# Spread in one tile width; token rows written early in three transfers, gates in a table of their own with a second gather per tile

## The reference, cut to what matters

```python
# _moe_ref: logits = x @ phi; slot_input = softmax_over_rows(logits).T @ x
slot_out[e] = relu(slot_input[e] @ w1[e]) @ w2[e]
x = softmax_over_slots(logits) @ slot_out          # comb @ slot_out
# _moe2_ref:
logits = x @ w_gate; e_idx = argmax(logits, axis=1)
gate_w = softmax(logits)[n, e_idx]
eom = sigmoid(x @ w_output_gate)
out[mask_e] = gate_w * eom[:, e] * (relu(x[mask_e] @ v1[e]) @ v2[e])
```

## Time and profile before

| | |
|---|---|
| median of 3 runs | 523.88 us (521.13 to 524.0) |
| profiled execution | 524.51 us, of it span 522.8 |
| mean granted TensorE clock | 0.959 |
| TensorE busy | 464.9 us, 89% of the span |
| L859, output products | 249.2 us |
| DMA queue of SP | 77.27 MB, 41.5% of 16 engines' time |

### The profile page before, as it was taken

The page is one execution under the profiler, slowest core; times in us unless marked ns, Lnnn a source line. Parts: engine busy times, 40 slices in busy tenths (PEclk is TensorE's granted clock), DMA queues, the critical chain, the costliest instruction groups (busy, mean ns, idle before and its releaser), DMA issues.

```text
span 522.8 us, 10083 instructions
## 1 busy us (share of the span) xinstructions
PE 464.9 (89%) x3524; PEld 253.7 (49%) x3525; DVE 135.9 (26%) x278; ACT 144.4 (28%) x330; POOL 139.4 (27%) x206
## 2 busy tenths in 40 slices
PE   4788886799847997889999999999999999999991
PEld 3567664553205444365454554554545545445440
DVE  1389899820000667110010110101101001011000
ACT  2587774301000343322121221211212212122110
POOL 2144433056000121402322323223233232232210
PEclk9999999899885798799999999999999999999997
DMA  8869736849999977876786101011011010110110
GB/s 253 278 228 322 260 101 230 319 173 369 387 390 409 396 270 291 257 239 192 243 291 222 44 26 46 26 43 43 26 46 43 26 46 23 45 43 23 41 42 2
DMA packets 42690, 88.35 MB, mean 169 GB/s; under 512 B 6142, under 2 KB 15362, under 8 KB 42656
## 3 DMA queue, kind: packets, MB, share of 16 engines
q1 hardware_dynamic: 37616, 77.27, 41.5%
q0 software_dynamic: 3952, 10.33, 5.9%
q10 hardware_dynamic: 1088, 0.26, 0.2%
HBM read 77.61 MB, written 10.59 MB: 169 GB/s over the span
## 4 chain that ended last, share of the span: by engine, by line
PE 78%; DVE 9%; DMA 4%; issue 3%; ACT 3%; SPq 0%; POOL 0%; DVEq 0%; POOLq 0%; ACTq 0%
PE bank L859 47%; DMA arena<-in_moe_w 4%; PE bank L848 3%; PE bank L847 3%; PE bank L722 3%; PE bank L523 3%; PE bank L740 2%; PE bank L515 2%; ACT parts L996 2%; PE bank L770 2%; PE bank L534 2%; DVE rsum L1103 1%; PE bank L787 1%; PE bank L789 1%; PE bank L788 1%
## 5 line engine op out<-in xcount | busy, mean ns | idle before, releaser
L859 PE MATMUL bank<-arena,z 128*128 x560 | 249.2, 598 | 1.0 <-DVE z L1367 0.8
L859 PEld LDWEIGHTS bank<-arena,z 128*128 128x128 f32 x560 | 103.6, 190 | 122.0 <-issue 119.9
L1367 DVE TENSOR_SCALAR z<-bank 128x512 f32<-128x512 f32 x35 | 24.2, 691 | 251.8 <-PE bank L848 251.8
L1034 ACT ACTIVATE z<-bank,tile_gate 128x512 f32<-128x512 f32 x35 | 24.0, 687 | 227.8 <-PE bank L859 227.8
L454 POOL COPY rows_to<-sidx 128x1 int32 (+1 forms) x35 | 6.3, 181 | 152.4 <-ACT z L1034 152.4
L462 POOL DMA_INDIRECT z<-token_rows,rows_from x36 | 37.9, 1054 | 29.0 <-POOL rows_from L454 29.0
L472 POOL DMA_INDIRECT out<-z,rows_to x35 | 35.7, 1019 | 29.9 <-POOL rows_to L454 29.9
L847 PE MATMUL bank<-cT,parts 128*128 128x128 bf16 x280 | 36.4, 219 | 0.5 <-issue 0.5
L848 PE MATMUL bank<-cT,parts 128*128 128x128 bf16 x280 | 36.5, 219 | 0.1
L847 PEld LDWEIGHTS bank<-cT,parts 128*128 x280 | 27.4, 98 | 1.2 <-issue 0.9
L848 PEld LDWEIGHTS bank<-cT,parts 128*128 x280 | 27.4, 98 | 1.0 <-issue 0.5
(11 more groups left out here) (223 smaller groups left out, 497.6 us busy)
## 6 DMA issues: line engine op xcount, KB each, us to landing
arena<-in_moe_w SPq DMA_DIRECT2D x31, 2048.0 KB, 11.6
arena<-in_x SPq DMA_DIRECT2D x8, 1024.0 KB, 7.2
parts<-in_moe_w SPq DMA_DIRECT2D x1, 2048.0 KB, 9.2
token_rows<-z SPq DMA_DIRECT2D x8, 162.0 KB, 3.2
z<-token_rows,rows_from POOLq DMA_INDIRECT x36, 2.6
out<-z,rows_to POOLq DMA_INDIRECT x35
z<-in_state ACTq DMA_DIRECT2D x4, 64.0 KB, 3.0
z<-in_state SPq DMA_DIRECT2D x4, 64.0 KB, 2.7
```

The source lines that it names most:

```text
L859: mm = e.matmul(pY[p][:, :], hT[p][:, c, :], arena[:, bass.ds(ex * UNIT + 512 * c, 512)], start=(c == 0), stop=(c == CF - 1))
L1034: e.activation(ysb[p], pY[p][:, :], ACT.Copy, scale=tile_gate[:, q:q + 1])\
L1367: e.tensor_scalar(hT[p][:, 4:8, :], bank[2 * p + 1][:, :].rearrange("p (c t) -> p c t", c=4), 0.0, None, ALU.max).then_inc(relu_v, 1)
```

## The change

- `spread` uses stationary operands of 64 columns throughout. `pick` has zeros in its outer two blocks, so that [I I], [I 0] and [0 I] can be cut from it; the upper half of banks 0 and 1 is a sum of two matmuls. 20 matmuls per expert in place of 16, 12 for banks 0 and 1 first, and a semaphore `spread_a` after them. ACT waits for `spread_a` for banks 0 and 1 and for `spread_psum` for banks 2 and 3; TensorE waits for ga_ready ahead of the first group and for gb_ready ahead of the second.
- The row table is 80 words wide and written after load 11 instead of load 20, in three DMAs of SP, as soon as GpSimd's copy is done.
- The gates go to a table of their own, by three DMAs issued by ACT after part_2(1). GpSimd gathers a tile's gates by a second indirect DMA into `tile_gate`; ACT's copy L1018 and its waits go.
- GpSimd's step is scatter(t), then gather(t+4) and gather_gate. The v2 loads of experts 0 and 1 no longer wait for gathers.

```diff
-            for u in range(8, 21):
+            for u in range(8, 12):
                 load_w(u)
-
-            e.wait_ge(row_ready, 2)
-            for b in range(NB):
-                e.dma_start(table[b * (S + NS):b * (S + NS) + S, :].rearrange("(p j) w -> p j w", j=J),
-                            rowbuf[:, J * b:J * b + J, :]).then_inc(table_out, 16)
-                q, f = b % 4, b // 4
-                e.dma_start(table[b * (S + NS) + S:(b + 1) * (S + NS), :],
-                            rowbuf[32 * q:32 * q + 32, NB * J + f, :]).then_inc(table_out, 16)
-            for u in range(21, NU):
+            e.wait_ge(row_ready, 1)
+            by_batch = table.rearrange("(b r) w -> b r w", b=NB)
+            e.dma_start(by_batch[:, 0:S, :].rearrange("b (p j) w -> p b (j w)", j=J),
+                        rowbuf[:, 0:NB * J, :].rearrange("p (b j) w -> p b (j w)", b=NB)).then_inc(table_out, 16)
+            for f in range(2):
+                e.dma_start(by_batch[4 * f:4 * f + 4, S:S + NS, :],
+                            rowbuf[:, NB * J + f, :]).then_inc(table_out, 16)
+            for u in range(12, NU):
                 load_w(u)
...
-                if ex < 2:
-                    e.wait_ge(gathers, 2 * ex + 2)
-                else:
+                if ex >= 2:
...
+            def gather_gate(q):
+                e.sem_inc(gate_turns, 1)
+                e.indirect_dma_start(tile_gate[:, q:q + 1], None, gates,
+                                     bass.IndirectOffsetOnAxis(ap=rows_from[:, q:q + 1], axis=0),
+                                     bounds_check=last_row, oob_is_err=False).then_inc(gate_in[q], 16)
...
             def step(t, q, first=False):
+                scatter(t, q, first and t < 2)
                 with live_tile(e, live, t + 4):
                     if not isinstance(t, int) or t + 4 < ST:
                         gather(t + 4, q)
-                scatter(t, q, first and t < 2)
+                        gather_gate(q)
...
-                gather(t, t, first=True)
+                gather(t, t)
+            e.wait_ge(gates_out, 16 * 3)
+            for t in range(4):
+                gather_gate(t)
...
                 if ex >= 1:
                     e.wait_ge(ga_ready, 2 * ex)
+                for q in range(4):
+                    at, cols = half(q)
+                    e.matmul(bank[q // 2][0:64, cols], at[:, 32:96], g1, start=True, stop=True)
+                    e.matmul(bank[q // 2][64:P, cols], at[:, 64:P], g1, start=True, stop=False)
+                    mm = e.matmul(bank[q // 2][64:P, cols], at[:, 0:64], g2, start=False, stop=True)
+                mm.then_inc(spread_a, 1)
+                if ex >= 1:
                     e.wait_ge(gb_ready, 2 * ex)
-                g1, g2, g3 = gp[ex % 2]
                 for q in range(4):
...
-                    e.matmul(ba[0:96, cols], at[:, 0:96], g1, start=True, stop=True)
-                    e.matmul(ba[96:P, cols], at[:, 0:32], g2, start=True, stop=True)
-                    e.matmul(bb[0:64, cols], at[:, 0:64], g2, start=True, stop=True)
-                    mm = e.matmul(bb[64:P, cols], at[:, 0:64], g3, start=True, stop=True)
+                    at, cols = half(q)
+                    e.matmul(bank[2 + q // 2][0:64, cols], at[:, 32:96], g2, start=True, stop=True)
+                    mm = e.matmul(bank[2 + q // 2][64:P, cols], at[:, 32:96], g3, start=True, stop=True)
                 mm.then_inc(spread_psum, 1)
...
+            e.wait_ge(gate_ready, 1)
+            by_batch = gates.rearrange("(b r) w -> b r w", b=NB)
+            e.dma_start(by_batch[:, 0:S, :].rearrange("b (p j) w -> p b (j w)", j=J),
+                        gate[:, 0:NB * J].rearrange("p (b j) -> p b j", b=NB)).then_inc(gates_out, 16)
+            for f in range(2):
+                e.dma_start(by_batch[4 * f:4 * f + 4, S:S + NS, :],
+                            gate[:, NB * J + f:NB * J + f + 1]).then_inc(gates_out, 16)
...
-                if not isinstance(t, int) or t > 3:
-                    e.wait_ge(y_copied, t - 3)
-                e.activation(tile_gate[:, q:q + 1], row[q][:, GATE_W:GATE_W + 1], ACT.Copy).then_inc(gate_saved, 1)
...
+                e.wait_ge(gate_in[q], 4 * (t - q) + 16)
...
-            e.wait_ge(row_ready, 1)
-            e.tensor_tensor(rowbuf[:, :, GATE_W], gate[:, :], st1[:, :], ALU.mult).then_inc(row_ready, 1)
+            e.tensor_tensor(gate[:, :], gate[:, :], st1[:, :], ALU.mult).then_inc(gate_ready, 1)
```

More of the change, by code:

```diff
@@ L40 @@
 UNIT = CD * F
-ROWW = 81
-GATE_W = 80
+ROWW = 80
 NOROW = 1 << 20
@@ L53, in last_user, with build @@
     return before[-1] if before else None
-def build(nc, x, state, phi, w1, w2, wgate, wogate, v1, v2, out, table):
+def build(nc, x, state, phi, w1, w2, wgate, wogate, v1, v2, out, table, gates):
     with ExitStack() as ctx:
@@ L221, in build @@
                                                        sem("sidx_ready"))
+        pick_zero = sem("pick_zero")
         pick_ready, table_out, row_zero = sem("pick_ready"), sem("table_out"), sem("row_zero")
@@ L229, in build @@
         y_psum, y_copied, from_copied, to_copied = sem("y_psum"), sem("y_copied"), sem("from_copied"), sem("to_copied")
-        gate_saved = sem("gate_saved")
+        gates_out, gate_in, gate_turns = sem("gates_out"), [sem(f"gate_in{q}") for q in range(4)], sem("gate_turns")
+        gate_ready = sem("gate_ready")
         turns, gathers, scatters = sem("turns"), sem("gathers"), sem("scatters")
@@ L390, in _ @@
             e.wait_ge(consts, 3)
+            e.memset(pick[:, :, :, :], 0.0).then_inc(pick_zero, 1)
+            e.wait_ge(pick_zero, 1)
             for q in range(4):
-                e.tensor_copy(pick[:, q, :, :], identb[:, 32 * q:32 * q + 32].unsqueeze(1)
-                              .to_broadcast([P, 4, NS])).then_inc(pick_ready, 1)
+                e.tensor_copy(pick[:, q, 1:3, :], identb[:, 32 * q:32 * q + 32].unsqueeze(1)
+                              .to_broadcast([P, 2, NS])).then_inc(pick_ready, 1)
             e.wait_ge(consts, 11)
@@ L446, in _ @@
             e.memset(z1[:, 0:4 * ROWW], 0.0).then_inc(row_zero, 1)
-            e.wait_ge(row_zero, 1)
-            e.wait_ge(table_out, 16 * 2 * NB)
+            e.memset(tile_gate[:, :], 0.0).then_inc(row_zero, 1)
+            e.wait_ge(row_zero, 2)
+            e.wait_ge(table_out, 16 * 3)
             last_row = e.to_reg(ROWS - 1)
@@ L455, in numbers, with gather @@
                 e.wait_ge(copied, t + 1)
-            def gather(t, q, first=False):
-                if not first:
-                    e.wait_ge(gate_saved, t - 3)
+            def gather_gate(q):
[3 more added lines that the diff above has]
+                                     bounds_check=last_row, oob_is_err=False).then_inc(gate_in[q], 16)
+            def gather(t, q):
                 numbers(rows_from[:, q:q + 1], t, from_copied)
@@ L778, in spread, with half @@
                 e.wait_ge(g3_done, ex + 1)
+                g1, g2, g3 = gp[ex % 2]
+                def half(q):
+                    at = pick[:, q, :, :].rearrange("p r s -> p (r s)")
+                    return at, slice(256 * (q % 2), 256 * (q % 2) + 256)
                 if ex >= 1:
                     e.wait_ge(ga_ready, 2 * ex)
+                for q in range(4):
[5 more added lines that the diff above has]
+                if ex >= 1:
                     e.wait_ge(gb_ready, 2 * ex)
-                g1, g2, g3 = gp[ex % 2]
                 for q in range(4):
-                    at = pick[:, q, :, :].rearrange("p r s -> p (r s)")
-                    ba, bb = bank[q // 2], bank[2 + q // 2]
-                    cols = slice(256 * (q % 2), 256 * (q % 2) + 256)
-                    e.matmul(ba[0:96, cols], at[:, 0:96], g1, start=True, stop=True)
-                    e.matmul(ba[96:P, cols], at[:, 0:32], g2, start=True, stop=True)
-                    e.matmul(bb[0:64, cols], at[:, 0:64], g2, start=True, stop=True)
-                    mm = e.matmul(bb[64:P, cols], at[:, 0:64], g3, start=True, stop=True)
+                    at, cols = half(q)
+                    e.matmul(bank[2 + q // 2][0:64, cols], at[:, 32:96], g2, start=True, stop=True)
+                    mm = e.matmul(bank[2 + q // 2][64:P, cols], at[:, 32:96], g3, start=True, stop=True)
                 mm.then_inc(spread_psum, 1)
@@ L992, in spread_out @@
             def spread_out(ex):
-                e.wait_ge(spread_psum, ex + 1)
+                e.wait_ge(spread_a, ex + 1)
                 for k in range(4 if ex < DVE_FROM else 2):
+                    if k == 2:
+                        e.wait_ge(spread_psum, ex + 1)
                     a = F * ex + 512 * (k % 2)
@@ L1392 @@
     table = nc.dram_tensor("token_rows", (ROWS, ROWW), F32, kind="Internal").ap()
-    build(nc, *args, out, table)
+    gates = nc.dram_tensor("token_gates", (ROWS, 1), F32, kind="Internal").ap()
+    build(nc, *args, out, table, gates)
```

1 line of the change is left out of this document (added).

## The result

| | before | changed |
|---|---|---|
| median | 523.94 us (4 runs) | 563.9 us (4 runs, 558.67 to 566.53) |
| profiled execution, its span | 524.51, 522.8 | 566.53, 564.7 |

The ratio is 1.0762, 95% interval 1.0674 to 1.085: slower by 40 us, where I had forecast 522.1 and a range up to 529.5.

A forecast was written before the change was run, and what follows sets the result against it. W2 was taken as bound by DMA bandwidth, the loop, over half the span, by TensorE; 4.2 - 3.4 - 4.5 - 0.1 + 2.0 = -1.8 gave a median of 522.1 us, range 516 to 529.5.

The forecast's parts named there:

- The loop: Loop of 35 tiles: period stays 8.07 us, extra gather hidden, rows landing with 1.0 us of slack; no steady cost.
- Rival 2: In the loop, the gather becomes the bound; from a landing of 3.7 us, one us per two tiles; 529 to 545; chance 0.13.
- The sum: All terms in the profiled execution: 4.2 - 3.4 - 4.5 - 0.1 + 2.0 = -1.8 us, giving 522.1 for the median.
- V2 loads over the first gathers: Early loop: ungated V2 loads delay about four gathers, +2.0 us, ends 0 and 4.
- W2: W2 stage, bound by DMA bandwidth: the earlier row table adds +4.2 us, ends +3.6 and +6.0.
- the 5.5: Gate table's time in us if a DMA's engine count divides the slowest dimension, 4 here; the forecast itself took nothing.
- The spread: Routing stretch: 20 matmuls of one width take 1.4 us instead of 2.7, in steps of 0.11 to 0.12.
- from the sort to the loop's first transpose: Between sort and loop: 15.3 to 17.6 us instead of 21.0 with the fast spread; a gain of 4.5 taken.
- The sort 3.4 earlier: Routing rounds: sort_rows comes 3.4 us earlier with the fast spread, ACT's DMA issues at 0.49 each adding no loss.
- the split: Routing rounds: ScalarE and TensorE may start on half the banks; overlap alone worth 0.5 us with the slow spread.
- Three issues in place of sixteen: SP's row-table writes: fewer issues are worth nothing by themselves, as SP isn't on the path.
- The ungated V2 loads: V2 loads of experts 0 and 1 start without the gathers' gate; the sum counts them as +2.0 us in the loop.

The follow-up runs named there:

- experiment 1: Changed kernel with the row gather back in its old place, ahead of the scatter, gate gather after it: 525.34 us, ratio 1.0035.
- experiment 2: Kernel before with scatter(t) moved ahead of gather(t+4) and nothing else: 555.34 us, ratio 1.0613.
- experiment 3: Changed kernel with both loads of the expert's number put ahead of TensorE's wait for rows in the looped tiles: 536.64 us.
- row-first run: Changed kernel with both gathers between the slot's output and its scatter, row gather ahead of gate gather: 531.14 us, ratio 1.0143.
- experiment 5: Changed kernel with both gathers between the slot's output and its scatter, gate gather ahead of row gather: 548.96 us, ratio 1.0466.
- experiment 6: On top of experiment 1, the three gate transfers issued by SP after load 20 instead of by ACT: 521.66 us, ratio 0.998.
- experiment 7: On top of experiment 1, the three row-table transfers put back behind load 20: 520.11 us, ratio 0.9966.
- experiment 8: Kernel before with only the one-width spread and its split semaphore: 516.79 us, ratio 0.9864.
- experiment 9: Kernel before with the one-width spread but without the split of the waits: 516.75 us, ratio 0.9833.
- experiment 11: On top of experiment 10, the late table, rows with gates, written in three transfers instead of sixteen: 512.48 us, ratio 0.9773.
- experiment 10: On top of experiment 8, the first two V2 loads no longer wait for gathers: 516.26 us, ratio 0.985.

## Why the prediction was wrong

**The loop, the step that failed.** I computed the row's slack as its landing against the array's transposes, 1.0 us, and held the steady loop to be free of cost. The number was right (the array started at 414.81, on time), the yardstick was wrong. Rival 2 had the place, the sign and the price of one us per two tiles for each us of landing, but put the start of it at a landing of 3.7. The sum and the rival both let the array begin when the rows land; neither has the sequencer's 3.9 us from its first load behind the wait to the output product. With them the cost starts at a lead of 2.9, which a gather that starts 3.6 before the array's need (411.20 for 414.81) and lands 2.6 later can't give, and it is 2.0 per two tiles at the 0.8 that is left, although nothing is late for the array. The trace of before held the evidence: at the start of its loop, where the sequencer isn't ahead, hidden(0) and hidden(1) follow at 0.14 and 0.11 per product, against 0.055 in the loop, and its two loads there are 2.7 apart:

```profile
L830 PEldq TENSOR_LOAD <-texp x2: 303/306/309, 228.3 to 231.0; - x2
```

I had used the 0.055 as the array's rate without asking what makes it possible. Size: after the first five intervals the loop takes 31.7 more, 5.1 of it in three products at the half clock, where the sum had nothing. Experiments 1 to 5.

**V2 loads over the first gathers.** Right in kind, mis-sized: the first five intervals take 9.8 more, where the sum had +2.0 for them. The cleaner figure is the 9.4 of the row-first run, in which the order costs nothing later; in both, two products at the half clock make 3.3 to 3.4 of it. With the gather in its old place the same early V2 loads cost nothing (loop 279.4 in experiments 1, 6 and 7).

**W2.** Right: +4.2 forecast, 3.2 to 3.4 measured; nearer to the 3.6 of the loads' own rate. The upper end was miscounted: 1.39 MB at the 212 GB/s of before are 6.6 and not 6.0. The trace has prices that I said or assumed it lacked: a packet of 1280 bytes takes 55 ns and not 65, one of the gates' 16-byte packets 9. The rule of the Trainium skill on the number of engines (DMA: Bandwidth & Descriptors; it stands under Why a DMA increments its semaphore by 16 and not by 1, not where the prediction names it) agrees with the trace: the 256 packets of state rows, 20 ns each, run between 135.82 and 137.12, which is the work of 3.9 engines. But the weight loads kept the rest busy (share 1.11, 384 GB/s in that stretch), so the 5.5 that I had from it did not come.

**The spread.** Right: 1.43 for 1.4, and 15.35 from the sort to the loop's first transpose, the lower end of my 15.3 to 17.6 (4.5 taken, 5.7 measured).

**The sort 3.4 earlier.** Wrong, +1.0. The term was ACT's DMA issues, 0.49 each from the earlier trace rows; in the saturated stretch they held ACT from 180.85 to 186.29. A price from the idle start of the kernel was carried to a place where DMA was at its limit. Experiment 6 gives 3.2 back; the sort then stands 2.4 nearer to W2's last group than before. Of the split I had expected an overlap; the medians of experiments 8 and 9 show none.

**Three issues in place of sixteen.** I held them to be worth nothing, since SP wasn't on the path. With the fast spread and a late table load 21 is on the path, behind these issues, and experiment 11 gains 2.7 to 3.8 by it. With the old spread no run tests it.

**The ungated V2 loads.** Counted only as a cost; experiment 10 shows no gain from them by themselves.

**The end, +2.9.** Not in the prediction at all.

## What to carry to other kernels

A wait in an engine's instruction stream has to be met before its sequencer gets there and not before its data path needs the operand: count the lead that the sequencer has in the present kernel, and the time from its first register load behind the wait to the last (here 2.9 us). A transfer's position relative to a wait on the same queue can matter more than its size; here one statement's order cost 32 us. The price of a DMA issue taken from an idle stretch need not hold where the DMA engines are at their limit (0.49 and 3.84 here).

## What the runs showed of the hardware

GpSimd's closing DRAIN is longer in the kernels that issued more indirect DMAs, though in the changed kernel the last of them had landed at 555.2, before it began. Before, and with the second gather:

```profile
L57 POOLq DRAIN  x1: 5873/5873/5873, 516.7 to 516.7; - x1
```

```profile
L56 POOLq DRAIN  x1: 8816/8816/8816, 555.6 to 555.6; - x1
```

71 indirect DMAs (36 gathers, 35 scatters) and 107: 83 and 82 ns each. All seven traces with 107 have 8813 to 8816 ns, all seven with 71 have 5873 to 5880. It accounts for the +2.9 of every kernel with the second gather. The dependence on the count is argued from two counts; no run varied it alone.
